# Lead of a fused attention and expert kernel: plain products for the first unit, one bias per pair, row-sum addition and zeros on ScalarE, other places for the splits of x

## What is computed

```python
def reference(...):
    attn_out = _attn_ref(q, k, v)     # 4 x 8 heads, 576 positions, head size 64
    x = attn_out.transpose(0, 2, 1, 3).reshape(B * S, H * D)      # 2304 x 512
    x = _moe_ref(x=x, **moe_kwargs)
    return _moe2_ref(x=x, **moe2_kwargs)
# _attn_ref: scores * scale + alibi bias, window of 128 behind the position, softmax
#            with attn / (sum + 1e-09), times v
# _moe_ref:  out += p[:, e:e+1] * (relu(x @ w1[e]) @ w2[e]) for 4 experts, hidden size 1024
# _moe2_ref: slots mixed from x by a softmax over tokens, 8 experts on 4 slots each,
#            combined by a softmax over slots
```

## Time and profile before

| | |
|---|---|
| median of 3 runs | 998.17 us (997.79 to 998.43) |
| profiled execution | 997.73 us, span 995.9 us, mean granted PE clock 0.982 |
| busy, share of the span | PE 96%, POOL 66%, DVE 60%, ACT 45% |
| lead, up to the last attention product outside the units | about 72 us |
| units | about 72 to 905 us |

### The profile page before, as it was taken

One profiled execution on the slowest core, in us unless ns is written; L12 is line 12 of the kernel. 1 busy time (PEld: TensorE's weight loads), 2 busy tenths in 40 slices (PEclk: granted clock), 3 DMA queues, 4 the chain that ended last, 5 costly groups with the idle time before them and its releaser, 6 DMA issues.

```text
span 995.9 us, 18516 instructions
## 1 busy us (share of the span) xinstructions
PE 957.9 (96%) x6067; PEld 793.7 (80%) x6067; DVE 596.0 (60%) x1175; ACT 446.6 (45%) x943; POOL 659.6 (66%) x587
## 2 busy tenths in 40 slices
PE   8879999999999989999999999989999999999896
PEld 6558888888888878888888888878888899887532
DVE  5895556565565776556566565665655656556602
ACT  4774444444444544444444444634434344432312
POOL 5988676667669796666667668797866676661000
PEclk8799999999999989999999999999999999999998
DMA  8633314214214213314214212119212122137896
GB/s 251 187 92 114 107 43 128 91 42 130 88 48 126 89 43 112 109 43 127 92 42 130 88 46 82 43 50 333 73 56 84 42 84 69 58 104 283 348 377 238
DMA packets 86403, 116.90 MB, mean 117 GB/s; under 512 B 6208, under 2 KB 56896, under 8 KB 86352
## 3 DMA queue, kind: packets, MB, share of 16 engines
q1 hardware_dynamic: 84736, 109.89, 33.9%
q0 software_dynamic: 1616, 6.36, 1.7%
HBM read 111.51 MB, written 4.72 MB: 117 GB/s over the span
## 4 chain that ended last, share of the span: by engine, by line
PE 82%; POOL 7%; DVE 4%; issue 4%; DMA 1%; ACT 1%; DVEq 0%; SPq 0%; POOLq 0%; ACTq 0%
PE banks L1364 36%; PE banks L1346 32%; PE banks L1304 3%; PE banks L1256 2%; POOL h_lo L665 2%; PE banks L1497 1%; PE banks L1524 1%; PE banks L1278 1%; POOL ws_lo L656 1%; PE banks L1280 1%; DVE w_lo L1043 1%; POOL w_lo L656 1%; PE banks L1237 1%; DMA out<-slot_w 1%; PE banks L1423 1%
## 5 line engine op out<-in xcount | busy, mean ns | idle before, releaser
L1071 DVE SCALAR_TENSOR_TENSOR acc<-banks,prob,acc 128x512 f32<-128x512 f32 x288 | 215.5, 748 | 191.4 <-PE banks L1364 191.2
L1364 PE MATMUL banks<-w_hi,h_hi 128*128 128x512 f32 x576 | 227.1, 394 | 5.0 <-POOL h_lo L665 2.7
L1364 PE MATMUL banks<-w_hi,h_lo 128*128 128x512 f32 x576 | 229.2, 398 | 0.0
L1364 PE MATMUL banks<-w_lo,h_hi 128*128 128x512 f32 x576 | 228.4, 396 | 0.0
L665 POOL TENSOR_TENSOR h_lo<-c,h_hi 128x384 fp32r<-128x384 f32 x144 | 149.8, 1057 | 103.4 <-ACT c L842 103.2
L840 ACT ACTIVATE h_hi<-c 128x384 fp32r<-128x384 f32 x144 | 75.0, 521 | 169.5 <-PE banks L1364 100.6
L656 POOL TENSOR_TENSOR ws_lo<-w_sum,ws_hi 128x1024 fp32r<-128x1024 f32 x48 | 117.0, 2438 | 33.4 <-ACT ws_hi L816 33.4
L1346 PE MATMUL banks<-xT_hi,ws_hi 128*128 128x384 f32 x384 | 131.3, 342 | 3.1 <-POOL ws_lo L656 3.1
L1346 PE MATMUL banks<-xT_lo,ws_hi 128*128 128x384 f32 x384 | 129.1, 336 | 0.0
L1346 PE MATMUL banks<-xT_hi,ws_lo 128*128 128x384 f32 x384 | 128.8, 335 | 0.0
L1364 PEld LDWEIGHTS banks<-w_hi,h_hi 128*128 128x128 f32 x576 | 108.7, 189 | 23.9 <-issue 9.2
(11 more groups left out here) (169 smaller groups left out, 1612.5 us busy)
## 6 DMA issues: line engine op xcount, KB each, us to landing
w_raw<-w SPq DMA_DIRECT2D x96, 512.0 KB, 4.1
slot_w<-m2w SPq DMA_DIRECT2D x4, 2048.0 KB, 11.9
v_b<-v_n SPq DMA_DIRECT2D x24, 256.0 KB, 5.4
slot_early<-m2w POOLq DMA_DIRECT2D x3, 2048.0 KB, 12.5
slot_early<-m2w SPq DMA_DIRECT2D x3, 2048.0 KB, 12.3
v_a<-v_n SPq DMA_DIRECT2D x20, 256.0 KB, 5.3
out<-slot_w SPq DMA_DIRECT2D x9, 512.0 KB, 4.7
q_b<-q_t SPq DMA_DIRECT2D x12, 288.0 KB, 4.6
```

The source lines that it names most:

```text
L1071: dve.scalar_tensor_tensor(acc[:, tile, :], ps_y[tt % 2][:, :], prob[:, tile, bass.ds(e, 1)], acc[:, tile, :], ALU.mult, ALU.add).then_inc ...
L1364: ins = pe.matmul(ps_y[tt % 2][:, :], hh[:, f, tt * P:(tt + 1) * P], wp[u % 2][:, f, :], start=m == 0, stop=m == 3 * FT - 1)
```

## The change

It has five parts. (1) The first unit's first layer is computed by plain products of x instead of the seven: four tiles of 384 columns (`PLAIN`), each over four heads' depth blocks with three matmuls each, 48 matmuls in place of 42. x is copied and split one head at a time, as each is finished (`x_head_hi` on ACT, `x_head_rest` on DVE); two tiles take their first three blocks in steps 24 and 25 of the lead, the remaining 30 matmuls follow it. The sums and ws_lo of the first unit's weights are not made. The parts T1 to T4 are needed from unit 1 on; POOL makes both halves, ACT copies and DVE splits them after the lead. (2) In the lead one bias is made for each pair instead of two. (3) The addition of 1e-9 to rsum goes from DVE to ACT, in the lead and in the body. (4) The zeros are written by ACT, six operations of 512 columns per pass. (5) In the transitions the copies and splits of x lie at other pieces, and the second bias of a pair at piece 41 instead of 30. PE's 46 transposes at the start become 8, and 42 more follow the scores of the first six steps (`FILL`).

The diff, cut to its core (left out: semaphore counts and buffer numbers that follow from it, and the two split functions, which are those of before on other slices):

```diff
+        FILL = {0: 4, 1: 12, 2: 8, 3: 8, 4: 6, 5: 4}
...
+            n = (v + 9) // ATT
+            return n if (v + 9) % ATT == 0 and 0 < n <= KD + 1 else None
...
-        X_HI_AT = [30, 32, 33, 35, 36, 38, 40]
-        ZERO_AT = 45
+        X_HI_AT = [29, 31, 33, 35, 37, 39, 41]
+        X_LO_AT = [30, 34, 35, 39, 39, 42, 43]
+        ZERO_AT = [46, 47, 48, 49, 50, 51]
...
+        PLAIN = [(0, 0), (1, 0), (0, 1), (1, 1)]
+        ps_plain = [bank[6], bank[7], bank[2], bank[1]]
+        T_ORDER = [1, 3, 4, 5]
...
-                if v == 6:
-                    w1_sums(0, 0, 0)
-                if v == 9:
+                if v == 8:
                     w1_rest(0, 0, 0, 0)
-                if v == 11:
-                    w1_rest(0, 0, 0, 1)
-                if v == 13:
+                    pool.wait_ge(s_w1lo, 1)
+                    pool.sem_inc(s_w1lo, 1)
+                if v == 14:
                     pool.wait_ge(s_oc, FROM + 4)
                     combine_x(0, slice(0, 1), 0)
-                if v in (16, 18, 20):
-                    x_rest(0, 0, v // 2 * 2 - 15, slice(0, 1))
-                if v == 21:
+                if v == 16:
                     w1_sums(0, 0, 1)
-            for n in (1, 3, 5):
-                x_rest(0, 1, n, slice(1, 2))
-            w1_rest(0, 0, 1, 0)
+                if v == 18:
+                    w1_rest(0, 0, 1, 0)
+            pool.wait_ge(s_oc, FROM + 2 * KD)
+            combine_x(0, slice(1, 2), 4)
...
-                            if t == 30 and (p + 2 < PASSES or not last):
-                                pair_bias(p + 2 if last else p + 1, n, 1)
+                                pair_bias(p + 2 if last else p + 1, n, 0, place(n, 0) - 3)
+                            if t == 41 and (p + 2 < PASSES or not last):
+                                pair_bias(p + 2 if last else p + 1, n, 1, place(n, 0))
...
-                            if last and t - 1 in X_HI_AT:
-                                n = X_HI_AT.index(t - 1)
-                                if n % 2:
-                                    x_rest(p + 1, p + 2, n, BOTH)
-                            if last and t == ZERO_AT:
-                                zero(p + 1)
+                                combine_x(p + 1, slice(1, 2), 4 * (2 * p + 3))
+                            if last and t in X_LO_AT[1::2]:
+                                x_rest(p + 1, 2 * X_LO_AT[1::2].index(t) + 1)
...
+                act.wait_ge(s_exp, FROM + place(n, a) + 1)
+                act.activation(rsum[:, a, :], rsum[:, a, :], ACT.Copy, bias=1e-9).then_inc(s_rplus, 1)
...
+            def zero(p, tt):
+                if p == 0:
+                    act.wait_ge(s_comb, 8)
+                    act.wait_ge(s_xlod, KD)
+                else:
+                    act.wait_ge(s_xlod, x_split_before(p + 1)[1])
+                    act.wait_ge(s_xlop, x_split_before(p + 1)[2])
+                act.activation(acc[:, p * NTP + tt, :], ident[:, 0:1].broadcast_to([P, D]), ACT.Copy,
+                               scale=0.0).then_inc(s_zero, 1)
...
+            plain_hi(0)
+            plain_hi(1)
+            t_hi(1)
+            plain_hi(2)
+            for tt in range(TT):
+                zero(0, tt)
+            plain_hi(3)
+            for tt in range(TT, NTP):
+                zero(0, tt)
+            for n in T_ORDER[1:]:
+                t_hi(n)
...
-                dve.wait_ge(s_exp, FROM + place(n, a) + 1)
                 dve.wait_ge(s_norm, FROM + place(n, a) - ATT + 1)
-                dve.tensor_scalar(rsum[:, a, :], rsum[:, a, :], 1e-9, None, ALU.add).then_inc(s_rplus, 1)
-                dve.wait_ge(s_rplus, place(n, a) + 1)
+                dve.wait_ge(s_rplus, FROM + place(n, a) + 1)
                 dve.reciprocal(rinv[:, a, :], rsum[:, a, :]).then_inc(s_rinv, 1)
...
+            plain_rest(0)
+            plain_rest(1)
+            dve.wait_ge(s_lo11, 1)
+            dve.wait_ge(s_lop, FROM + 1)
+            dve.sem_inc(s_u, 4)
+            x_rest(0, 1)
+            plain_rest(2)
+            dve.wait_ge(s_lop, FROM + 2)
+            dve.sem_inc(s_u, 1)
+            plain_rest(3)
+            for n in T_ORDER[1:]:
+                x_rest(0, n)
             for p in range(PASSES):
-                dve.wait_ge(s_zero, p + 1)
+                dve.wait_ge(s_zero, NTP * (p + 1))
...
+            def plain(i, ks):
+                f, b = PLAIN[i]
+                for k in ks:
+                    pe.wait_ge(s_xlod, HEADS.index(k) + 1)
+                    kk, n = k % 2, k // 2 * 2 + 4 * b
+                    w_hi, w_lo = [w[0][:, k, f * P:(f + 1) * P] for w in (w1_hi, w1_lo)]
+                    for m, (w, x) in enumerate(((w_hi, xT_hi), (w_hi, xT_lo), (w_lo, xT_hi))):
+                        ins = pe.matmul(ps_plain[i][:, 0:TB], w, x[:, kk, n, :],
+                                        start=k == HEADS[0] and m == 0, stop=k == HEADS[-1] and m == 2,
+                                        skip_group_check=True)
+                if ks[-1] == HEADS[-1]:
+                    ins.then_inc(s_mm1, NPROD - 3 if i == 3 else 1)
...
-            keep_warm(46, bank[1])
+            keep_warm(8, bank[5])
             pe.wait_ge(s_zrow, 4)
             for v in range(FIRST, LEAD):
                 j = v + LEAD_S
                 if 0 <= j < LEAD:
                     scores(*step(j), True)
+                if j in FILL:
+                    keep_warm(FILL[j], bank[5])
                 if v in (LEAD - 3, LEAD - 2):
                     pe.wait_ge(s_neg, FROM + LEAD)
-                    product(0, 0, 0, v - LEAD + 3, (0,))
+                    pe.wait_ge(s_w1lo, 2)
+                    plain(v - LEAD + 3, HEADS[:-1])
...
-            for n in range(NPROD):
-                product(0, 0, 0, n, (1,) if n < 2 else (0, 1))
+            for i in range(4):
+                plain(i, HEADS[-1:] if i < 2 else HEADS)
```

More of the change, by code:

```diff
@@ L651, in w1_rest @@
                 i = u % 2
-                pool.wait_ge(s_w1hi, 2 * unit(p, e, u) + part + 1)
+                first = isinstance(e, int) and unit(p, e, u) == 0
+                pool.wait_ge(s_w1hi, 2 if first else 2 * unit(p, e, u) + part + 1)
                 if part == 0:
@@ L751, in expert @@
                             hid_rest(*up, 2)
-            for j in range(3):
-                hid_rest(0, 0, 0, j)
             for p in range(PASSES):
@@ L777, in _ @@
         def _(act):
[L778 removed]
+            for s_x in (s_exp, s_oc, s_rplus):
                 act.sem_inc(s_x, FROM)
+            act.sem_inc(s_u1, 1)
             def exps(p, n, a, lead):
@@ L1005, in mask_min @@
                 w = width(p, a)
-                late = a // 3
+                mine = bias[bias_buf(n, a, lead)]
                 c0 = BAND if is_first(p, a) else 0
@@ L1009, in mask_min @@
                 dve.wait_ge(s_exp, FROM + place(n, a) - 1)
-                dve.wait_ge(s_bias, 2 * n + late + 1)
+                dve.wait_ge(s_bias, bias_no(n, a, lead))
                 dve.nop(nofuse=True)
@@ L1015, in mask_min @@
                         in0=ps_s[:, h, 0:w],
-                        in1=bias[late][:, h, c0:c0 + w], scale=-SCALE, scalar=3e38,
+                        in1=mine[:, h, c0:c0 + w], scale=-SCALE, scalar=3e38,
                         op0=ALU.add, op1=ALU.min, accum_out=negmax[:, a, h:h + 1])
@@ L1339, in product @@
+                if isinstance(e, int) and e == 0 and u == 0:
+                    x_ready(p, n)
+                if p == 0 and u == 1 and n in T_ORDER:
+                    pe.wait_ge(s_xlod, KD + T_ORDER.index(n) + 1)
+                for kk in range(2):
                     q = W_AT_N[n]
```

208 lines of the change are left out of this document (101 added, 107 removed).

## The result

The changed kernel takes 985.36 us (median of 4 runs, 984.1 to 986.76), before 998.3 (4 runs: the three of the table above and 999.4); the ratio is 0.9872, 95% interval 0.9855 to 0.989. The forecast was 984.0, the range 978.5 to 990.5. The profiled execution took 986.28 us, 11.45 less than that of before.

The account below looks back on a forecast made before the run. PE was taken as the bound except in the lead and two transitions. Gains of 10.5 (transitions), 2.4 (lead) and 1.0 (hand-over) made 13.9 us, from 997.73 profiled to 984.0 us, range 978.5 to 990.5.

Parts of the forecast that it names:

- The reading of before: Transitions: POOL's bias delays ws_lo, and DVE's addition and splits delay acc and h_lo; idle PE and half clock cost 12.3 us.
- the 9.5 that was named as a sign: First transition: PE busy over 9.5 of 10 us and a clock of 1.0 would show the prediction right.
- only its last link can shrink: Second transition: no bias there, so POOL's chain shortens only in ws_lo; first gap of 1.5 us shrinks to 0.6 to 1.5.
- Its own sign of being wrong: Transitions: the prediction is wrong if either still shows half clock.
- The rival of half the price: Transitions: ws_lo still comes after the PE, since DVE's splits lock POOL; gain 5 instead of 10.5, 989.5 us; 16 in 100.
- (a): Start of the lead: fewer transposes first, but k_b's load caps it; product of 26.31 at 24.7 at the earliest, 1.6 us gained.
- (b): Lead: POOL gives out the last norms; three xT_lo and one bias off, one w_lo on, 1.9 us less.
- (e): Lead: ACT takes 27 additions to rsum at 0.33 us, 8.9 in all, without being the bound; the chain changes little.
- (d): Lead: DVE loses 27 additions (10.6 us busy) and has room for its splits; two long operations now adjacent, counted at nothing net.
- the rival that the lead doesn't warm up: Lead: with 8 transposes the clock stays at half until about 20 us; 5.6 us worse, 990; 12 in 100.
- The hand-over: Lead's end to third second-layer group: six products fewer, but PE waits 1.3 us for ACT; net 1.0 us gained.
- The forecast's rule on the shared port: VectorE and GpSimd lock each other out at their port pair, ScalarE is free; DVE's new splits would lock POOL out.

Follow-up runs that it names:

- five splits on DVE: Changed kernel with POOL's first split of x in the transitions (for product 1) given to DVE at piece 32: 982.39 us, ratio 0.9853 to before.
- the changed kernel's second profile: The changed kernel run again with nothing altered, beside the others on one chip, and profiled again: median 985.45 us.
- both edits: Changed kernel with the split for product 1 on DVE and the expert probabilities moved in the lead: four steps later 981.21 us, in step 5 982.61.
- the three parts undone: Changed kernel with the addition on DVE, old places of x's copies and splits, and bias at piece 30, zeros still on ACT: 994.70 us.

## Why the forecast was right, and where it wasn't

**The transitions, first.** The reading of before is confirmed in the main. The 1.6 us for ws_lo are the bias's (put back, 1.60 returned). The gap of h_lo and acc, and the half clock behind it, are the splits' first of all: with only their old places put back there is one gap of 2.94 and the clock falls; with only the addition back on DVE there are three gaps of 0.55 to 0.57 and it doesn't. But the shares were not what the working suggested: it dwelt on the bias and on DVE's 2.32 us, and the old places, put back alone, cost 4.8 of the 6.0. The forecast allowed for 6.7, with 0.3 us of waiting left; 0.88 are left, so PE is busy 9.12 of 10 us there and not the 9.5 that was named as a sign.

**The transitions, second.** This is the term that was mis-sized, 3.8 for a measured 1.5. The step was "only its last link can shrink: 3.36 against the mean of 2.44 if DVE's split no longer runs beside it". It ran beside it, with w_lo ahead of it (3.35 us, as before), and the first gap stayed at 1.52 where I had taken 1.1; the second kept 0.57 of its 2.32 where I had said that it goes. Then the clock fell, at 1.3 us, which the forecast had counted as gained. Its own sign of being wrong, half clock in either transition, is there. The rival of half the price was thus right in this transition and wrong in the first. That POOL's order was the cause is shown by the kernel with five splits on DVE.

**The lead.** 3.2 for 2.4. (a) The product that I put at 24.7 at the earliest stands at 25.12 in the changed kernel, behind a wait for k_b, so 1.2 of the 1.6 us were gained there. But 24.7 was no bound: in the other kernels it stands at 23.5 to 25.1, since k_b lands between 22.2 and 24.2, and in three of the thirteen, the changed kernel's second profile among them, the PE doesn't wait for k_b just before it. Whether this term reaches the end of the lead isn't shown. (b) POOL's shorter list, 1.9 us: not measured as it stands. Four biases put back cost 2.1, but the term was one bias and three splits off and one w_lo on. (e) ACT's addition takes 0.204 us, where I had 0.26, or 0.33 with its wait; put back on DVE it cost 0.3 us in the hand-over. So the lead's 3.2 us aren't parted into these terms, and that its sum came near is no proof of them. (d) Two of DVE's other long operations following each other, "which I count at nothing net", brought a wait of 1.97 us and half clock to 46.8. Before had half clock in that place as well (37.9 to 48.1), so the net isn't known. A fall of the clock before 25 us, the sign of the rival that the lead doesn't warm up, is in no profile of a changed kernel; the earliest are at 25.2 and 26.0, in the two kernels with both edits.

**The hand-over.** 1.4 for 1.0; all profiles have 14.4 to 14.8 us. The PE's wait for ACT's first product of unit 1, which the forecast put at 1.3 us, is the 0.59 shown above.

**Left out.** The forecast had no term for what comes behind the transitions. At the start of the third pass POOL issues the loads of the last stage, and a load of weights takes up to 9.9 us to land. Before, the longest took 9.3. POOL's timeline has the wait for the transfer:

```profile
683.67 0.74 POOL L663 TENSOR_TENSOR w_sum<-w_raw 128x256 f32<-128x256 f32 x1 [5.67 <-DMA w_raw<-w]
```

And h_lo, queued behind, is late for the PE:

```profile
693.57 0.49 PE L1435 MATMUL banks<-w_hi,h_hi 128*128 128x512 f32 x1 [0.64 <-POOL h_lo L688]
```

It costs 0.55 us more than before here. Over all profiles the stage goes with the landing: 31.87 us with 9.4 in the changed kernel's second profile, 32.3 to 32.5 with 9.8 to 10.0, 33.2 with 10.7 to 11.4 in four others (addition on DVE, 46 transposes, both edits, two biases). Since the changed kernel alone has 32.33 once and 31.87 once, how much of this is the change's and how much chance isn't known; nor is why the load takes longer, and an order that keeps it ahead of the others wasn't tried.

That the sum was near is in part luck, because errors partly cancel: 1.2 us more than forecast in lead and hand-over, 3.0 less in the transitions and 0.55 lost behind them. The gain is 11.45 us for 13.9, and the median lies 1.4 us above the forecast.

## What to carry to other kernels

Where two engines share a list of splits, count for each stretch what stands on each ahead of the one result that the PE wants next: moving one split of 2.6 us from POOL to DVE took 1.1 us off each transition, and 1.3 more off the second where the clock had fallen, while the bias's new place was worth 1.5 in one, the addition 1.0 and the zeros nothing. Measure the parts of a kernel as stages between fixed instructions of the PE: the transitions repeat within 0.1 us, but for a fall of the clock, where medians of one kernel scatter by 1. Profile a kernel twice before reading a wait or a stage from it: the waits for POOL's pr in the lead were 0.2 and 2.9 us in two profiles of one kernel. Look at the stage behind a shortened one too: 0.55 us of what was gained here ended there in one profile, in a wait for a transfer, and 0.1 in the other.

## What the runs showed that I hadn't expected

The clock's fall after a gap isn't settled by the gap: 1.5 and 0.57 us of idle time led to half clock in the second transition of four profiled executions and not of four others, at 1.2 to 1.3 us each time. Where the second gap was 2.3 us (five transitions: both of before and of the three parts undone, and the second with the old places), or one gap 2.94 (the first with the old places), the clock fell each time; where the first transition had only gaps of 0.53 to 0.57 us and 0.32 to 0.34, never.

The same addition on two columns takes ACT 0.204 us on the mean of 72, and DVE 0.27 to 0.30 on the mean, but 2.32 in one place and 0.97 in another when POOL is busy. In the same way POOL's ws_lo takes 2.46 us on the mean, and 3.1 to 3.4 beside DVE's w_lo and splits. The forecast's rule on the shared port (the Trainium skill, SBUF — State Buffer, Who interferes with whom) fits these rows, and so does the second half of its warning: a split that goes to DVE makes operations of POOL beside it longer, 1.46 us for a sum instead of 0.73 and 4.65 for three h_lo instead of 3.66. That is less than the 2.58 that it takes off POOL's own list.
